# Where VectorE multiplies the probabilities by 1/sum in the rounds of a windowed attention

## The reference, cut to what matters

```python
# per (batch, head); q, k, v are 576 x 64
q_d, k_d, v_d = (a.reshape(144, 4, 64).mean(1) for a in (q, k, v))
out_up = np.repeat(softmax(q_d @ k_d.T / 8) @ v_d, 4, axis=0)
mask = abs(i - j) < 4                                   # 7 keys for each query
out_local = softmax(where(mask, q @ k.T / 8, -1e9)) @ v
x = out_up + out_local                                  # 1152 tokens x 512
e = argmax(x @ w_gate); gate = softmax(x @ w_gate)[e]
y = gate * (relu(x @ w1[e]) @ w2[e])                    # at most 288 tokens an expert
h = y @ w_in; out = (h * tanh(softplus(h))) @ w_out
```

## Time and profile before

| | |
|---|---|
| median of 3 runs | 483.32 us (481.43 to 490.93) |
| the profiled execution | 488.61 us, span 486.5 us |
| PE, DVE, ACT, POOL busy | 93%, 57%, 47%, 28% |
| rounds 0 to 18 | 10 to 116 us of the span |
| TensorE's clock, mean over the span | 0.966 of full speed |

### The profile page before, as it was taken

One profiled execution on the slowest core, in us unless ns is written; L12 is line 12 of the kernel. 1 busy time (PEld: TensorE's weight loads), 2 busy tenths in 40 slices (PEclk: granted clock), 3 DMA queues, 4 the chain that ended last, 5 costly groups with the idle time before them and its releaser, 6 DMA issues.

```text
span 486.5 us, 10257 instructions
## 1 busy us (share of the span) xinstructions
PE 454.6 (93%) x3520; PEld 420.3 (86%) x3521; DVE 275.3 (57%) x660; ACT 229.3 (47%) x629; POOL 134.9 (28%) x133
## 2 busy tenths in 40 slices
PE   9756899988879999999999999999999999999993
PEld 8645798778779999999999988899999888899982
DVE  5575647878211111011111399888888888888883
ACT  2653467860312333233224366665655565765541
POOL 8484332412000000000000565433352223443202
PEclk9876999997989999999999999999999999999998
DMA  9969898412558799897775314231232121141001
GB/s 186 190 117 170 156 369 287 154 66 101 194 173 293 265 348 328 276 328 268 269 243 188 121 44 83 48 87 44 88 108 86 43 80 50 54 142 43 1 0 65
DMA packets 72001, 74.87 MB, mean 154 GB/s; under 512 B 32800, under 2 KB 47776, under 8 KB 71968
## 3 DMA queue, kind: packets, MB, share of 16 engines
q1 hardware_dynamic: 70240, 69.71, 48.4%
q0 software_dynamic: 1728, 4.72, 2.5%
HBM read 64.98 MB, written 9.44 MB: 153 GB/s over the span
## 4 chain that ended last, share of the span: by engine, by line
PE 85%; DVE 8%; issue 2%; ACT 2%; DMA 1%; POOL 0%; POOLq 0%; SPq 0%; ACTq 0%; DVEq 0%
PE ps L1097 79%; PE ps L1173 1%; PE ps L1312 1%; DVE pr L893 1%; PE ps L1116 1%; PE ps L1168 1%; PE ps L1108 1%; DVE qT L854 1%; DMA xg<-x_by_expert 1%; DMA x_by_expert<-x_sb,xslot 1%; DVE sme L888 1%; PE ps L1218 0%; ACT pr L663 0%; ACT prT L646 0%; DVE kdT L840 0%
## 5 line engine op out<-in xcount | busy, mean ns | idle before, releaser
L597 POOL TENSOR_TENSOR wiL<-raw,wiH 128x512 fp32r<-128x512 f32 x48 | 62.4, 1302 | 259.5 <-ACT wiH L646 156.1
L1097 PE MATMUL ps<-hid,raw 128*128 128x128 f32 (+2 forms) x512 | 72.3, 301 | 3.4 <-issue 3.4
L1097 PEld LDWEIGHTS ps<-hid,raw 128*128 128x128 f32 x512 | 70.4, 195 | 3.6 <-issue 3.6
L1097 PE MATMUL ps<-xe,raw 128*128 128x128 f32 (+2 forms) x512 | 70.3, 298 | 1.4 <-issue 0.8
L1097 PEld LDWEIGHTS ps<-xe,raw 128*128 128x128 f32 x512 | 68.8, 191 | 2.3 <-issue 1.4
L1097 PE MATMUL ps<-x2L,wiH 128*128 128x384 f32 x192 | 65.3, 340 | 0.0
L1097 PE MATMUL ps<-x2H,wiH 128*128 128x384 f32 x192 | 65.1, 339 | 0.2 <-DVE x2L L1013 0.2
L1097 PE MATMUL ps<-x2H,wiL 128*128 128x384 f32 x192 | 64.6, 337 | 0.0
L1097 PE MATMUL ps<-woH,gH 128*128 (+1 forms) x144 | 56.9, 395 | 1.9 <-DVE gL L1013 1.9
L1097 PE MATMUL ps<-woH,gL 128*128 (+1 forms) x144 | 57.1, 397 | 0.0
L1097 PE MATMUL ps<-woL,gH 128*128 (+1 forms) x144 | 56.7, 394 | 0.0
(11 more groups left out here) (130 smaller groups left out, 770.7 us busy)
## 6 DMA issues: line engine op xcount, KB each, us to landing
raw<-in_moe_w SPq DMA_DIRECT2D x32, 1024.0 KB, 6.4
raw<-in_moe_w_in SPq DMA_DIRECT2D x24, 512.0 KB, 3.7
x_by_expert<-x_sb SPq DMA_DIRECT2D x1, 4608.0 KB, 15.8
xg<-x_by_expert SPq DMA_DIRECT2D x8, 512.0 KB, 3.7
wo_in<-in_moe_w_out SPq DMA_DIRECT2D x8, 512.0 KB, 7.4
v<-in_v SPq DMA_DIRECT2D x4, 576.0 KB
qk_tok<-in_k SPq DMA_DIRECT2D x8, 256.0 KB, 4.4
qk_tok<-in_q SPq DMA_DIRECT2D x8, 256.0 KB, 5.0
```

What stands on the lines that cost most here:

```text
L597: nc.gpsimd.tensor_tensor(wiL[:, r, :, :], raw_wi_tile(r), wiH[:, r, :, :].bitcast(F32), ALU.subtract).then_inc(s_wil, 1)
L1097: return T.matmul(out_, a, b, start=start, stop=stop, skip_group_check=True)
```

## The change

In each round VectorE does `norm(n-1)` first, ahead of `stats(n)` and of `q_copy(n+2)`. Nothing else in any queue changes, and the same instructions run with the same operands.

```diff
             for n in range(ROUNDS):
+                if 0 <= n - 1 < NS:
+                    norm(n - 1)
                 if n < NS:
                     stats(n, count_turn(n))
                 if turned(n) is not None:
                     q_copy(turned(n))
-                if 0 <= n - 1 < NS:
-                    norm(n - 1)
                 if count_turn(n) is not None:
                     if n >= NS:
                         read_counts(count_turn(n))
```

## The result

The median of 20 executions is 479.88 us (476.62 to 485.09), against 485.80 us (481.43 to 491.21) for 20 of the kernel before: 5.9 us less. The ratio, without the executions that lie more than 1.5% above the fastest of their kernel, is 0.991, 95% interval 0.988 to 0.994: 4.5 us, or 0.9%. The forecast had 471.5 and a gain of 12. The time lay at the upper edge of the range, and the gain was at most half of what I had forecast. Executions of one kernel differ here in the mean granted clock of TensorE, and their times with it; that turns out to be the main point.

What follows compares the result with a forecast made beforehand. PE, busy 93%, was taken as the bound, losing time waiting for norm's product (11.1 us) and to the slow clock that follows. Gains 12.2 + 1.0 less 1 gave 12.2 us, 471.1 to 476 by median; forecast 471.5, range 465 to 480.

Steps and rivals of the forecast that it cites:

- Rounds 1 and 2: First attention rounds: maxima at 17.4 and 21.7 us; step 1's transposes start at 21.7, were at 27.54, 5.8 us won.
- the walk: Early attention rounds re-timed in the new order with profiled durations: 15.0 us won by round 7, 12.2 with some slow clock.
- Round 3: norm(2) runs under GpSimd's sums, taken at half the difference between 1.15 and 2.52 us; maximum at 27.3, was 32.73.
- Round 4: First down step: dummies start 7.1 us earlier; a clock drop to 1.2 GHz costs rounds 4 and 5 2.8 us more.
- Rounds 5 to 7: The 3.7 us wait and slow matmuls behind it vanish; round 7 starts 15.0 us earlier, 12.2 with the clock drop.
- The sign of being wrong: In the profile after: PE waiting for a load or for pooled tiles, among the listed signs that the prediction failed.
- Rounds 13 and 14: Late local rounds, with waits of 0.51 us on PE and 0.73 on VectorE: 0.5 us won each, 1.0 together.
- Behind the attention: Everything behind round 14: instruction order as before, no gain counted.
- The median: Whole kernel: how much of 12.2 us comes off the median 483.32; 471.1 in full, 476 if faster executions have less to win.
- that rival: Whole kernel: gain cut to 6 to 8 us by late vwin or fast executions without slow clock; 475 to 477.5, chance 0.34.
- rival 1: Rounds 2 to 6 keep 2.4 GHz: 15.0 + 1.0 us off the median, 467.5; chance 0.18.
- The slower rival: Local rounds: exponentials, norm and maximum form one 4.5 us chain; nine steps lose 10.3 us, 493.7; chance 0.02.

Runs made afterwards that it cites:

- a2: The changed kernel, unedited, profiled a second time; median 481.64 us, ratio 0.993 to the kernel before.
- e_late: Changed kernel with norm of steps 0 to 4 back behind the maximum, only steps 5 to 14 ahead of it; 486.63 us, ratio 1.005.
- x4: Changed kernel plus 66 dummy matmuls in PE's waits of rounds 3, 4 and 7; 470.39 us, ratio 0.970 to the kernel before.
- b5: The kernel before, unchanged, in another profiled execution, a fast one; span 480.0 us, mean clock 0.984.
- b4: The kernel before, unchanged, in another profiled execution; span 482.1 us, mean clock 0.977.
- x3: Kernel before, old order, plus 146 dummy matmuls in PE's waits of rounds 1 to 4 and 7; 482.30 us, ratio 0.996.

## Why the prediction was wrong

- *Rounds 1 and 2*: right. The maxima came 4.82 and 9.24 us behind that of step 0 (17.92 and 22.34, from 13.10); the walk had 4.8 and 9.1. The new wait for the exponentials showed (0.79 and 0.80 us on VectorE), and left PE idle for 0.79 and 0.55 us, close to the walk's 0.5 and 0.4.
- *Round 3*: `norm(2)` took 2.58 us, not the 1.8 in between. *Round 4*: the clock fell in that round, as taken (16 dummies in 2.29 us), but the transposes of round 5 ran at full speed again (1.04 us). The slow stretch cost about 1.5 us and not 2.8.
- *Rounds 5 to 7*: 12.3 us at the start of round 7 against 12.2, `attend` of step 0 at 54.55 in the range of 52 to 55, `vwin` at 33.7 and waited for by nobody. Against the trace on which it rests, the walk was right. That it is right to 0.1 us is partly luck: the two misses above go against each other, and this trace ran 0.5 us late from the start (step 0's maximum at 13.10, before 12.59).
- *The sign of being wrong* that did show was PE's wait for `pooled`: 3.2 us, it had been 1.8. It is behind these waits that a2 lost its clock, in rounds 4 and 7.
- *Rounds 13 and 14*: 1.0 us forecast, about 0 measured. From step 10 to the expert rows it takes 43.2 to 44.0 us before and 42.8 to 43.4 after, and e_late is 0.5% slower as a whole, which I cannot place: its trace is 0.9 us shorter in that part.
- *Behind the attention* I had taken nothing. From the expert rows to the feed-forward it is 157.2 to 159.5 us before and 158.5 to 159.8 after: no difference that one can tell.
- *The median*: this is the step that failed. It saw that the profiled execution lay 5.3 us above the median of three, and named the mechanism, faster executions with less slow clock to win back. Then it gave that rival 0.34 and put the forecast at nearly the full 12.2 us off the median. The runs show that the clock goes with most of the spread of before (mean span 487.3 us at a clock under 0.97, 479.4 at 0.985 and above). Of the 12.2 us only about 5 are there in each execution. The 7 that were clock exist against the slower executions alone, and the changed kernel loses as much clock on average, 23.1 us at 1.2 GHz against 22.6, in waits of its own: round 3's, the one for pooled tile 4, the one for pooled tile 8. x4 fills these three. Its 15.5 us are near the 16 of rival 1, by luck: about 4 of them come from expert 0.
- *The starting point*: the median of three, 483.32, was 2.5 us below that of 20, so of the 8.4 us between forecast and measured time 2.5 were there from the start, and 5.9 are gain that did not come.
- *The slower rival* did not come: the chain of exponentials, `norm` and maximum sets the pace of round 2 at 4.4 us (17.92 to 22.34), near the 4.5 that it said, but that is less than the 7.3 and 9.5 us of before.

## What to carry to other kernels

A trace is one execution. Where part of the cost is the clock, look at the mean clock of the timed executions first, price the waits at full clock, and count the clock only as far as the new order leaves no wait of like length. In this kernel the order that removed idle time from TensorE also kept more of the clock only once the waits that remained were filled: it was worth 0.9% alone and 2.6% with 66 dummies in three waits. The version with both, 470.4 us, is the best one run, 3.0% below the kernel before; part of that, about 4 us, is the shorter standstill in expert 0 and the clock kept there, which no change to the attention was meant to touch.

## What was not expected of the hardware

- Like idle times end differently. 2.02 us ahead of round 1's transposes were followed by 1.2 GHz in the first trace, while b5 stood idle for 2.15 us at the same place and kept 2.4 GHz. In round 7 a2 lost the clock behind 2.02 us, while b5 and b4 kept it behind 1.93 and 2.05. The rows of b5, where the 12 and 16 dummies run at full clock:

```profile
18.55 1.04 PE L1173 MATMUL ps<-cst,pr 128*70 128x128 f32 x8 [2.15 <-DVE pr L893]
19.43 0.99 PE L1097 MATMUL ps<-warmb 128*128 128x160 bf16 x12
...
49.93 1.27 PE L1097 MATMUL ps<-warmb 128*128 128x160 bf16 x16 [1.93 <-DVE kdT L840]
```

- The length of TensorE's queue ahead of the loop over the experts sets how long the loop's first pass stands still: 3.5 us, 7.2 with 146 matmuls more (one kernel), 0.7 to 0.9 with 66 more, in two places and with either order. The part of the kernel in which that lies differs by 8 us between x3 and x4 (162.4 and 154.4), more than the whole of the change is worth, so kernels that differ in this length are not to be compared for a gain of this size.
